# A fused attention, channel-mix and mixer kernel on one core: the first tokens' loads, splits and softmax steps in another order

## What is computed

```python
# q, k, v: (4, 8, 576, 64)
scores = (q @ k.transpose(0, 1, 3, 2)) / 8.0
# heads 0-3: 0 <= rel < 32;  heads 4-7: 0 <= rel < 128 and rel % 4 == 0   (rel = query - key)
attn = softmax(where(mask, scores, -1e9)); attn_out = attn @ v
x = attn_out as (4, 576, 512)
# channel mix, d_ff = 1024
xk = mu_k * x + (1 - mu_k) * x_prev;  xr = mu_r * x + (1 - mu_r) * x_prev    # x_prev: one token back
x = sigmoid(xr @ w_r) * (relu(xk @ w_k) ** 2 @ w_v)
# mixer
u = x + token_mlp(x);  out = u + relu(u @ w_ch1) @ w_ch2
```

## Time and profile before

| | us |
|---|---|
| median of 3 runs | 794.73 (794.71 to 795.23) |
| the profiled execution, its own time | 796.07 |
| the profiled execution, span from first to last instruction | 794.2 |

### The profile page before, as it was taken

The page is one execution under the profiler, slowest core; times in us unless marked ns, Lnnn a source line. Parts: engine busy times, 40 slices in busy tenths (PEclk is TensorE's granted clock), DMA queues, the critical chain, the costliest instruction groups (busy, mean ns, idle before and its releaser), DMA issues.

```text
span 794.2 us, 15659 instructions
## 1 busy us (share of the span) xinstructions
PE 745.8 (94%) x6616; PEld 719.5 (91%) x6616; DVE 387.8 (49%) x594; ACT 256.9 (32%) x636; POOL 238.7 (30%) x242
## 2 busy tenths in 40 slices
PE   4788999999999999999987999999999999999997
PEld 3577999999898989999976999999999999999997
DVE  5737876767577776768677121341215212251211
ACT  2445454453535354445341111321114111241111
POOL 5848474564746464555145000000000000000000
PEclk9998999999999999999998999999999999999999
DMA  8811312321221212020451000120001100010001
GB/s 204 242 31 40 66 49 45 72 45 41 58 50 35 58 29 48 17 60 1 166 212 60 1 1 2 37 84 1 1 1 60 61 1 1 1 61 1 2 1 59
DMA packets 67796, 39.80 MB, mean 50 GB/s; under 512 B 55119, under 2 KB 59023, under 8 KB 67727
## 3 DMA queue, kind: packets, MB, share of 16 engines
q1 hardware_dynamic: 65583, 34.09, 16.3%
q0 software_dynamic: 1088, 4.72, 1.7%
q10 hardware_dynamic: 1056, 0.00, 0.1%
HBM read 29.36 MB, written 4.72 MB: 43 GB/s over the span
## 4 chain that ended last, share of the span: by engine, by line
PE 79%; POOL 8%; DVE 5%; issue 3%; ACT 3%; DMA 1%; SPq 0%; ACTq 0%; DVEq 0%; POOLq 0%
PE bank L602 13%; PE bank L603 12%; PE bank L604 12%; PE tq L602 4%; PE tq L604 4%; PE tq L603 4%; PE bank L526 3%; PE bank L1003 3%; PE s L1003 3%; PE s L1001 3%; PE bank L1002 3%; PE bank L1001 3%; PE s L1002 3%; PE bank L497 3%; PE s L422 2%
## 5 line engine op out<-in xcount | busy, mean ns | idle before, releaser
L602 PE MATMUL bank<-xk_hi,WK_hi 128*128 128x288 f32 x256 | 80.9, 316 | 11.3 <-ACT kr L648 7.5
L602 PE MATMUL bank<-k_hi,WV_hi 128*128 128x288 f32 x256 | 78.3, 306 | 0.0
L977 DVE SCALAR_TENSOR_TENSOR h_lo<-tq,h_hi 128x288 fp32r<-128x288 f32 x48 | 22.0, 458 | 115.3 <-ACT h_hi L973 115.3
L977 DVE SCALAR_TENSOR_TENSOR h_lo<-bank,h_hi 128x288 fp32r<-128x288 f32 x48 | 21.9, 458 | 114.6 <-ACT h_hi L973 114.6
L666 POOL TENSOR_TENSOR k_lo<-kr,k_hi 128x288 fp32r<-128x288 f32 x64 | 56.7, 890 | 67.8 <-ACT k_hi L662 67.8
L603 PE MATMUL bank<-xk_hi,WK_lo 128*128 128x288 f32 x256 | 76.7, 300 | 0.0
L604 PE MATMUL bank<-xk_lo,WK_hi 128*128 128x288 f32 x256 | 76.5, 299 | 0.0
L603 PE MATMUL bank<-k_hi,WV_lo 128*128 128x288 f32 x256 | 75.5, 295 | 0.0
L604 PE MATMUL bank<-k_lo,WV_hi 128*128 128x288 f32 x256 | 75.3, 294 | 0.0
L652 DVE TENSOR_TENSOR kr<-kr 128x288 f32<-128x288 f32 x64 | 45.1, 705 | 42.0 <-ACT kr L648 41.2
L826 POOL DMA_DIRECT2D xcur<-X x4 | 3.2, 800 | 204.8 <-DVE U L935 187.6
(11 more groups left out here) (142 smaller groups left out, 2239.1 us busy)
## 6 DMA issues: line engine op xcount, KB each, us to landing
C_raw<-in_moe_w_ch SPq DMA_DIRECT2D x6, 1024.0 KB, 11.0
qraw<-in_q SPq DMA_DIRECT2D x24, 192.0 KB, 3.4
kraw<-in_k SPq DMA_DIRECT2D x24, 192.0 KB, 4.0
xcur<-X POOLq DMA_DIRECT2D x4, 1152.0 KB, 6.2
out_x<-ost SPq DMA_DIRECT2D x16, 240.0 KB, 2.6
vt<-in_v SPq DMA_DIRECT2D x44, 80.0 KB, 2.4
vt<-in_v SPq DMA_DIRECT2D x8, 320.0 KB, 3.3
WK_raw<-in_moe_w_k SPq DMA_DIRECT2D x4, 512.0 KB, 6.2
```

Source lines behind the costliest of these rows:

```text
L602: e.matmul(out_ap, wh, xh, start=start and i == 0, stop=False)
L977: e.scalar_tensor_tensor(lo, ps, 0.0, hi.bitcast(F32), ALU.max, ALU.subtract).then_inc(Z.h2l_done, 1)
```

## The change

It touches the prologue, and one line pair in the products that follow.

- The first k is issued by ScalarE's queue, ahead of the two small transfers of `mu`, while SyncE issues the first q.
- The second pair of tiles (tiles 2 and 3) gets buffers of its own, `qraw1`, `kraw1`, `vt2`, `vt3`, laid where `k2` will be later, so that its loads wait for nothing; `w_r` and `w_v` are loaded after them.
- `split_wk`: `hi` moves from VectorE to ScalarE, `lo` from GpSimd to VectorE. In the list the eight pieces go 0, 2, 3, 3 to iterations 0 to 3 (before: two each), and they stand behind `weighted_values(n - 1)` and ahead of `sums(n)`.
- `scores(n + 1)` comes ahead of `p_transpose(n - 1, 1)`; `sums(n)` and `normalise(n)` come ahead of `x_evict(n - 1)` and the differences; in iteration 3 `mix(0, 0, 0..1)` and `mix_parts(0, 0, 0..1)` come ahead of `split_wr(0..1)`.
- TensorE waits for the identity alone (`const_done` 3), and its list begins with `warm_up()`: 16 float32 matmuls of 128x128 by 128 columns on the identity, into a bank that nobody reads.
- In the products: the square reads the bank again, `max(ps, 0) * t`, in place of `t * t`, and the product that reuses the bank waits for the square (`sq_done`) in place of the relu (`relu_done`).

```diff
 def split_wk(i):
-    def vector(e):
+    def scalar(e):
         e.wait_ge(wk_in[i // 2], 16)
-        e.tensor_copy(hi, raw).then_inc(Z.wk_hi, 1)
-    def gpsimd(e):
+        e.activation(hi, raw, ACT.Copy).then_inc(Z.wk_hi, 1)
+    def vector(e):
         e.wait_ge(Z.wk_hi, i + 1)
         e.tensor_tensor(lo, raw, hi.bitcast(F32), ALU.subtract).then_inc(Z.wk_lo, 1)
...
+qraw1, kraw1, v2, v3 = [at(n, [P, 1024], F32, k2_offset + 4096 * m) for m, n in enumerate(("qraw1", "kraw1", "vt2", "vt3"))]
...
 def load_qk(s):
     def sync(e):
+        if s > 1:
+            e.wait_ge(Z.tq_done, 2 * s if s > 2 else 2)
+        load_rows(e, s, q, q_dst, q_landed)
+        if s:
+            if s > 1:
+                e.wait_ge(Z.tk_done, 2 * s if s > 2 else 2)
+            load_rows(e, s, k, k_dst, k_landed)
...
 def load_v(n):
     def sync(e):
-        wait(e, Z.o_done, n - 1)
+        if n >= 4:
+            e.wait_ge(Z.o_done, n - 1 if n >= 6 else n - 3)
...
 def bank_free(e, hh, kind, i):
     if k_ == "k":
-        e.wait_ge(Z.relu_done, FT1 * hh + n + 1)
+        e.wait_ge(Z.sq_done, FT1 * hh + n + 1)
...
 def up(hh, f):
     def vector(e):
         e.wait_ge(Z.relu_done, j + 1)
-        e.tensor_tensor(t, t, t, ALU.mult).then_inc(Z.sq_done, 1)
+        e.scalar_tensor_tensor(t, ps, 0.0, t, ALU.max, ALU.mult).then_inc(Z.sq_done, 1)
...
+def warm_up():
+    def tensor(e):
+        for _ in range(16):
+            e.matmul(mlp_ps[0][:, 0:P], ident[:, :], ident[:, :], start=True, stop=True)
...
 def prologue():
-    steps = loads() + [transposes(0), evictions(0), scores(0)]
+    steps = loads() + [warm_up(), transposes(0), evictions(0), scores(0)]
     for n in range(AHEAD + 1):
...
         steps += [mask_max(n)] if run_ else []
-        steps += [p_transpose(n - 1, 0)] if old else []
         steps += [evictions(n + 1)] if more else []
         steps += [subtract_max(n)] if run_ else []
+        steps += [p_transpose(n - 1, 0)] if old else []
+        steps += [scores(n + 1)] if more else []
         steps += [p_evict(n - 1, 0), p_transpose(n - 1, 1)] if old else []
-        steps += [split_wk(2 * n), split_wk(2 * n + 1)] if run_ else []
         steps += [exponentials(n)] if run_ else []
         steps += [p_evict(n - 1, 1)] if old else []
-        steps += [scores(n + 1)] if more else []
-        steps += [weighted_values(n - 1), x_evict(n - 1)] if old else []
+        steps += [weighted_values(n - 1)] if old else []
+        if run_:
+            steps += [split_wk(i) for i in ((), (0, 1), (2, 3, 4), (5, 6, 7))[n]]
+        steps += [sums(n), normalise(n)] if run_ else []
+        steps += [x_evict(n - 1)] if old else []
         if n == AHEAD - 1:
             steps += [difference(0, 0), difference(0, 1)]
-        steps += [sums(n), normalise(n)] if run_ else []
-        if n == AHEAD - 1:
+            steps += [mix(0, 0, 0), mix(0, 0, 1), mix_parts(0, 0, 0), mix_parts(0, 0, 1)]
             steps += [split_wr(0), split_wr(1)]
-            steps += [mix(0, 0, 0), mix(0, 0, 1), mix_parts(0, 0, 0), mix_parts(0, 0, 1)]
...
 @block.scalar
+    load_first_k(e)
...
 @block.tensor
-    e.wait_ge(Z.const_done, 9)
-    e.wait_ge(Z.zeroed, 1)
+    e.wait_ge(Z.const_done, 3)
```

More of the change, by code:

```diff
@@ L104, in build @@
         WV, o = weights("WV", [P, FT1 * DM], o)
+        k2_offset = o
         k2, o = split("k2", [P, FT1 * HALF], o)
@@ L315, in where, with raws, values, load_rows @@
             return s // NSU, s % NSU, dil
+        def raws(s):
+            if s == 1:
+                return (qraw1, Z.q_in_1, 32), (kraw1, Z.k_in_1, 32)
+            rank = s - (s > 1)
+            return (qraw, Z.q_in, 32 * (rank + 1)), (kraw, Z.k_in, 32 * (rank + 1))
+        def values(n):
+            if n in (2, 3):
+                return (v2, v3)[n - 2], (Z.v_in_2, Z.v_in_3)[n - 2], 16 * v_loads(n)
+            return vts[n % 2], v_in[n % 2], 16 * sum(v_loads(m) for m in range(n % 2, n + 1, 2) if m not in (2, 3))
+        def load_rows(e, s, src, dst, landed):
+            b, j, _ = where(2 * s)
+            for u in range(2):
+                e.dma_start(dst[0:2 * QB, DM * u:DM * (u + 1)].rearrange("p (h d) -> p h d", d=D),
+                            src[b, :, SU * j:SU * (j + 1), :].rearrange("h (m u) d -> u m h d", u=2)[u]).then_inc(landed, 16)
         def load_qk(s):
-            b, j, _ = where(2 * s)
+            (q_dst, q_landed, _), (k_dst, k_landed, _) = raws(s)
             def sync(e):
[L322 to L327, removed]
+                if s > 1:
[5 more added lines that the diff above has]
+                    load_rows(e, s, k, k_dst, k_landed)
             return dict(sync=sync)
+        def load_first_k(e):
+            dst, landed, _ = raws(0)[1]
+            load_rows(e, 0, k, dst, landed)
         def v_loads(n):
@@ L356, in load_v @@
             return dict(sync=sync)
-        def v_landed(n):
-            return 16 * sum(v_loads(m) for m in range(n % 2, n + 1, 2))
         def transposes(n):
@@ L365, in tensor @@
             def tensor(e):
-                for g, (raw, landed, done, read) in enumerate(((qraw, Z.q_in, Z.tq_done, Z.q_done), (kraw, Z.k_in, Z.tk_done, Z.k_done))):
-                    e.wait_ge(landed, 32 * (n // 2 + 1))
+                for g, (source, done, read) in enumerate(zip(raws(n // 2), (Z.tq_done, Z.tk_done), (Z.q_done, Z.k_done))):
+                    raw, landed, count = source
+                    e.wait_ge(landed, count)
                     wait(e, read, n)
@@ L514, in weighted_values @@
         def weighted_values(n):
-            vt = vts[n % 2]
+            vt, landed, count = values(n)
             def tensor(e):
                 e.wait_ge(Z.ptb_done, n + 1)
-                e.wait_ge(v_in[n % 2], v_landed(n))
+                e.wait_ge(landed, count)
                 wait(e, Z.x_done, n)
@@ L737, in flat @@
             return [s for u_ in units for s in u_]
+        def warm_up():
+            def tensor(e):
+                for _ in range(16):
+                    e.matmul(mlp_ps[0][:, 0:P], ident[:, :], ident[:, :], start=True, stop=True)
+            return dict(tensor=tensor)
         def prologue():
-            steps = loads() + [transposes(0), evictions(0), scores(0)]
+            steps = loads() + [warm_up(), transposes(0), evictions(0), scores(0)]
             for n in range(AHEAD + 1):
-                more, run_, old = n + 1 < AHEAD, n < AHEAD, 1 <= n <= AHEAD
+                more, run_, old = n + 1 < AHEAD, n < AHEAD, 1 <= n
@@ L761, in prologue @@
             return steps + [difference(0, 2), difference(0, 3), mix(0, 0, 2), mix(0, 0, 3), mix_parts(0, 0, 2), mix_parts(0, 0, 3)]
         def loads():
-            steps = [load_qk(0), load_v(0), load_v(1), load_weights1(w_k, WK, 0, 1, wk_in[0]), load_qk(1),
+            steps = [load_qk(0), load_v(0), load_v(1), load_qk(1), load_weights1(w_k, WK, 0, 1, wk_in[0]),
                      load_weights1(w_k, WK, 1, 1, wk_in[1]), load_weights1(w_k, WK, 2, 1, wk_in[2]),
-                     load_weights1(w_k, WK, 3, 1, wk_in[3]), load_weights1(w_r, WR, 0, 4, Z.wr_in), load_v(2),
-                     load_weights1(w_v, WV, 0, 4, wv_in[0]), load_weights1(w_v, WV, 4, 4, wv_in[1]), load_v(3), load_qk(2)]
+                     load_weights1(w_k, WK, 3, 1, wk_in[3]), load_v(2), load_v(3), load_weights1(w_r, WR, 0, 4, Z.wr_in),
+                     load_weights1(w_v, WV, 0, 4, wv_in[0]), load_weights1(w_v, WV, 4, 4, wv_in[1]), load_qk(2)]
@@ L1129, in _ @@
             for t, w in zip(kTs, (WINDOW + S, WINDOW + SUB)):
-                e.memset(t[:, :].rearrange("p (r x) -> p r x", x=w)[:, :, 0:WINDOW], 0.0)
+                last = e.memset(t[:, :].rearrange("p (r x) -> p r x", x=w)[:, :, 0:WINDOW], 0.0)
+            last.then_inc(Z.zeroed, 1)
             for t in vts:
```

11 lines of the change are left out of this document (5 added, 6 removed).

## The result

The changed kernel takes 798.3 us (median of 7 runs, 797.49 to 799.5), against 794.83 for the kernel before on the same chip: a ratio of 1.0040 (95% interval 1.0029 to 1.0052), 3.5 us slower. The forecast was slower by 8.2. The sign and the chain of the prologue were right; the size was not.

What follows compares the result with a forecast made beforehand. Dependent steps, tile by tile, were taken to bound the prologue until 49.26 us, then TensorE. Terms 1.2 - 0.9 + 3.6 + 2.6 + 1.7 = +8.2 us gave 802.9 us, range 795.5 to 807.

Steps and rivals of the forecast that it cites:

- the term of the products: Products after the prologue: holding the bank until the square is done delays a product in five half batches, +1.7 us.
- The rival that GpSimd is relieved: Products at 65 to 70 us: less GpSimd work closes TensorE's waits, the clock does not fall at 68; 798.3 us, 15%.
- The start: Prologue up to the first mask: 16 warm-up matmuls delay q's transposes, partly regained by a higher clock, +1.2 us.
- Tile 0: Prologue, tile 0 from mask to normalised: add and subtract no longer slowed by GpSimd's WK_lo and casts, -0.9 us.
- Tiles 1 to 3: Prologue, between normalises: sums wait behind WK_lo, WK_hi and an eviction, 8.2 then 8.8 us a tile, +3.6 us.
- The tail: Prologue's end: tile 3's evictions wait on ScalarE behind two xk_hi and two WR_hi, +2.6 us.
- The rival of the clock that holds through the prologue: Prologue: warm-up keeps TensorE's clock at the upper level until the products begin; 795.7 us, 12%.
- The two dear rivals: Start: warm-up matmuls cost 0.54 us each, 806.6 us, 8%. Products: bank held at full price, 808.9 us, 8%.

Runs made afterwards that it cites:

- e5: Kernel before with only the two lines of the products changed (square reads the bank, bank free after the square): 792.52 us, ratio 0.9969.
- e9: Kernel before with only the wait changed (bank free after the square), square still t*t from SBUF: 800.18 us, ratio 1.0065.
- e3: Changed kernel with sums(n) and normalise(n) ahead of split_wk: 794.73 us, ratio 0.9993.
- e8: Changed kernel without warm-up, first k on SyncE, tail as in e7, split_wk cut in two with sums behind no split: 787.46 us, ratio 0.9903.
- e2: Changed kernel with the two lines of the products as before (square t*t, bank free after the relu): 800.40 us, ratio 1.0066.
- e6: Changed kernel without the 16 matmuls and with the first k on SyncE's queue behind q: 796.54 us, ratio 1.0018.
- e4: Changed kernel without the 16 warm-up matmuls: 798.04 us, ratio 1.0036.
- e7: Changed kernel with mix_parts(0, 0, 0..1) and split_wr(0..1) moved behind the evictions of tile 3's probabilities: 795.36 us, ratio 1.0008.

## Why the prediction was right or wrong

**The step that failed is the term of the products**, +1.7, with its bounds -1 to +4.7. It measured -2.5 (e5). I had found the right wait (a product of each later half batch waits for the square, 1.67 us) and priced the hold rightly in kind: alone it costs 0.52 in a half batch in which the clock stays up (e9). What I left at nothing, though I wrote in the rivals that it could be more, is the other half of the same line: a square that reads the bank runs in 0.45 us however busy GpSimd is, and GpSimd's subtract and normalise beside it end 0.07 us sooner on average, and 0.22 sooner in the one place that decided (1.48 before by the timeline at 204 us, 1.26 after). The row that I cited for it, 0.447 against 0.705, was counted as relief "off the path", when the chain of that half batch ran through both: with the change it is 0.69 shorter than with the hold alone. That is -0.17 four times and -0.40 once, 1.06 in all, in place of +0.35 five times. The larger part, 1.4, is the first half batch, below.

**The rival that GpSimd is relieved**, at 15%, came nearest: it said 798.3, by the clock that doesn't fall. It took 4.6 off the sum; the products measured 4.2 below their term. But that it names the measured time to the tenth is luck, and its mechanism is half right. Near 68 us the clock stayed up in all seven traces with the edit of the products (the change and e3 to e8), and fell behind the wait of 2.2 us in both traces of before and in e2. (I had put that fall behind two waits; the timeline of before has the wait of 2.20 ahead of it, at 66.93, and the one of 1.60 behind it.) It fell in e2 although the eight `WK_lo` were gone from GpSimd, and it stayed up in e9, where no square read the bank: by these traces what kept it up there is the hold, which cuts the wait up, and not a faster GpSimd. How much of the 1.4 of the first half batch is the clock is open: no run held the clock and left the rest, and the moment at which it rises after the restart, between 3.4 us (e2) and 5.6 us (the change, the first trace of before), moves that half batch by about a microsecond as well (68.89 in e6, where it rises after 3.7, and 69.76 in the change, from the restart to the first gate product of the second).

**The start**, +1.2: +0.37 in the profiled execution. In the traces of kernels with the warm-up the first mask came at 10.78, 11.01, 12.82 and 12.82, as the 16 matmuls took from 5.19 to 6.75 us, depending on when the clock rose in them. So the term lies between 0.4 and 2.4, and 1.2 is inside. At the lower level they cost 0.42 us each (6.72 for 16, nearly all of them at that level), as I took (0.41). The estimate from the Trainium skill's FP8 and Floating Point Precision, TensorE Precision Notes (four passes, 0.43), agrees with it as well. What I priced at nothing, the second queue, costs 1.5 us by itself (e6 against e4); with the warm-up q's transposes stand behind the 16 matmuls until 6.92 or later, and it hardly shows. The warm-up itself wins nothing over its absence (e4).

**Tile 0**, -0.9: -0.96. **Tiles 1 to 3**, +3.6: +2.91. The first two were right to 0.1 (8.12 and 8.74 between normalises against 8.2 and 8.8); the third took 8.2 where I had 8.8: there is no tile 4 in the prologue, so the 1.28 of its scores drops out of that chain, and TensorE waits 0.72 for an eviction in its place. e3 shows the cause: without the order of sums and splits 4.5 us of the 25.07 vanish.

**The tail**, +2.6: +2.26, and e7 takes it all back. The differences took 1.28 us as no split ran beside them (before, `WR_lo` on VectorE), in place of 1.74.

**The rival of the clock that holds through the prologue** is refuted: 0.50 from 12 to 58 us. **The two dear rivals** are refuted as well, though the second's price for the hold was near the truth without the bank read (e9, +5.2).

The clock rose within the 16 matmuls and was back at 1.2 GHz by 12 us. Of the Trainium skill's two rules in TensorE: Matmul & The Clock Gate, the one in What's actually happening, by which activity releases the throttle, agrees with the rise, and the one in Part 4: PE-mode transpose, by which transposes do not count as busy in the same way, with the loss; but scores and idle time lay there too, and no run tells them apart.

In sum: of 8.2 forecast, the prologue's 6.5 measured 4.6 at the restart of the profiled execution, 6.65 at that of e2 (55.91, the same prologue with the late mask) and 5.3 in time (e2), and the products' +1.7 measured -2.5.

## What to carry to other kernels

When a step is moved ahead of another on an in-order engine, ask what the moved step waits for: here two splits that wait for a third engine stood ahead of the softmax sums, and each tile paid for the whole detour; the same work behind a step whose result is not awaited (the next maximum) let the tiles stand 5.0, 6.9 and 5.7 us apart in place of 8.1, 8.7 and 8.2 and, together with the tail in another order and without the warm-up and the second queue, turned +3.5 us into -7.7 (e8). An edit that holds a buffer longer and makes its reader faster must be priced as two terms and measured as two, for here they were +5.2 and about -7.7 (the second is a difference, -2.5 less +5.2, and both hold what the clock did). Where a second queue makes the transfers together no faster, issue them in the order in which they are needed, not at once (here 1.5 us).

## What the runs showed of the hardware that I had not expected

- A VectorE operation with one operand in PSUM took 0.45 us beside a busy GpSimd (64 squares, 405 to 460 ns), the same with both in SBUF 0.45 to 1.5 us; and GpSimd's operations beside it were 6% shorter on average.
- Between the rise near 54 us and 400 us the clock fell to 1.2 GHz only behind single waits of TensorE of 2.2 us or more (once in each trace of before and in e2, twice in e9), and not always behind those (e9 has five of 2.30 or 2.31). It then stayed at the lower level for 6.8 us in both traces of before and for 3.4 in e2 and e9. It stayed up in the kernels whose longest wait there was 1.7 us, though three waits close together summed to more (0.48 + 1.64 + 1.05 in e5). One more fall, shortly after 400 us, is in the change as in the kernel before (mean granted clock 0.87 from 400 to 440 us in both).
- k on a second queue made q land 1.5 us later (7.1 against 5.6), while all transfers together moved 216 and 213 GB/s from 3 to 6 us.
- The record of the granted clock shows 1.00 until its first change, also where the matmuls' durations tell of the lower level: before the first rise the durations are the better witness.
